# Chunked recurrence on one Trainium2 core: a new order of TensorE's groups within a chunk, a reordered prologue, and transfers that are merged, moved and split

## The chip, the cores and the metric

The kernel runs on one core of one Trainium2 chip. The metric is the device time of one execution in microseconds (us), here the median of several runs.

## The reference

Three parts follow one another: a recurrence over 768 steps for 4 batches x 8 heads with head dimension 40, a mixture of 8 experts (top 2), and a two-layer network. The change lies in the recurrence, and in the zeros that the routing needs in its sorted buffer.

```python
for t in range(S):                        # S = 768, state [B, H, 40, 40]
    y[:, :, t] = einsum('bhd,bhde->bhe', rt, state)
    Sa = einsum('bhde,bhe->bhd', state, at)
    state = state * wt[:, :, None, :] - einsum('bhd,bhe->bhde', Sa, bt)
    state = state + einsum('bhd,bhe->bhde', vt, kt)
x = attn_out as [3072, 320]
... top-2 routing: out[mask] += top2_w * (relu(x[mask] @ w1[e]) @ w2[e])
... h = x @ w_in; out = max(0.01 h, h) @ w_out
```

## The kernel before

The 768 steps are cut into 6 super-chunks of 128 steps (index s) and 24 chunks of 32 (index k = 4s + c, so c runs over 0 to 3). Everything of the recurrence is one unrolled program in `stage_a`, with the order of each engine written out by hand and semaphores between the engines. Stages for routing, experts and the last two layers follow and are not touched.

Per super-chunk: VectorE scans the reversed decays P to suffix products (`suffix`, L302) and the decays U to prefix products (`prefix`, L312); GpSimd multiplies A, B and K by them (`make_A`, `make_B`, `make_K`); TensorE forms two matrices per chunk, `lb` (L561) and `lk` (L571); ScalarE copies their diagonal blocks to LbS and LkT (`gram`). The LbS blocks go through DRAM (`lscr`) into lanes, Lt; VectorE solves a triangular system in 31 steps of a multiply (L331) and a reduction (L335), in `inverse`, a generator whose steps are spread over the chunks: 14 for c = 0, 12, 18, and the rest for c = 3. The result goes through DRAM (`tscr`) into TT. `decay` (L344) carries the state from one super-chunk to the next, behind the inverse in VectorE's order, and `y_out` (L357) of chunk k-2 stands ahead of chunk k's steps; it waits for p_y, which the last group of `add_K` raises.

Per chunk TensorE runs groups, in this order before: `first` (L533, X from the state), `gram_of(0)` (an `lk` or `lb` for a later super-chunk), `turn_S` (L599), `grow_K` (L632), `solve` (L609, needs TT), `gram_of(1)`, `read_S` in two halves (L623), `turn_P` (L614), `add_B` (L651), `tok`/`rows` (L582, L584 and L590, L592), `grow_B` and `add_K` in alternating halves (L642, L661), `gp` (L668), then for the next chunk `lkv` (L543) and `gv` (L554). `read_S`, `add_B` and `add_K` work on the output of the chunk before. ScalarE copies each result out of PSUM (its `copy` helper is L406): Xs, GvT, S0, PTs, Pn, S0T, Gpb; GpSimd masks GvT and Gpb.

SyncE's queue (SP) carries the wide inputs of a super-chunk (P, AT, BT, KT, each about 835 KB, `wide`), U (`decays`), and the ways through DRAM (`out_half`, `to_lanes`, `from_lanes`, `to_blocks`, the last with 16 transfers). ScalarE's queue loads each chunk's RT, VT and Vd two chunks ahead (`chunk`, six transfers) and stores the rows of the result. Vd is block-diagonal: its zeros are written once by GpSimd, each load fills four blocks of rows of 160 B. GpSimd starts one transfer of 9920 KB that fills `xsort` with zeros from xT (L273).

## Time and profile before

| | us |
|---|---|
| median of 3 runs | 1630.61 |
| lowest, highest | 1625.28, 1632.7 |
| the profiled execution, its own time | 1626.74 |
| its span in the trace | 1625.0 |
| TensorE busy (81%) | 1313.9 |
| VectorE busy (57%) | 921.0 |
| ScalarE busy (40%) | 653.4 |
| GpSimd busy (19%) | 315.4 |

The mean granted TensorE clock is 0.87 of full speed. In the trace an engine's busy time counts its compute instructions; "idle before" with an arrow names what ended the idle time, and "issue" means that the profile shows nothing that was waited for. Rows of a timeline begin with the start in us from the start of the span and the length.

### The profile page before, as it was taken

Reading aid. Unit: us, or ns where it says so; the run is one execution under the profiler, and the core shown is the slowest. Engines: PE = TensorE matmul, PEld = TensorE weight load, DVE = VectorE, ACT = ScalarE, POOL = GpSimd, SP = SyncE. Lnnn points to the kernel's source line nnn. Section 1 sums busy time; section 2 is a strip of 40 time slices with the busy share of each in tenths; the row PEclk is TensorE's granted clock in tenths of the full one; section 3 lists DMA queues with packets and bytes.
Section 4 is the critical chain, followed back from the end, with each engine's and each line's share of the span. In section 5 each row is a group of like instructions: output and inputs, shape, how many; then the busy total and the mean of one; then the engine's idle time right before and its main releaser. Section 6 shows DMA issues by size and latency. Waiting matters only on the chain. (4 is left out here: it accounts for less than half of the span.)

```text
span 1625.0 us, 40719 instructions
## 1 busy us (share of the span) xinstructions
PE 1313.9 (81%) x16814; PEld 1194.8 (74%) x16814; DVE 921.0 (57%) x1547; ACT 653.4 (40%) x1451; POOL 315.4 (19%) x255
## 2 busy tenths in 40 slices
PE   0546869798789895005999999999993999999998
PEld 0435758586677684005999999999993889889887
DVE  4575939555683502505777877777772453544533
ACT  0422434334344232204666666766661333323332
POOL 1332425241332110660000000000003210110000
PEclk9985877758687876557999999999996999999999
DMA  8577272624532212736667677677662110110000
GB/s 182 116 245 167 57 154 55 156 66 94 136 76 57 57 49 87 245 121 212 217 222 253 212 231 246 210 241 237 207 207 61 45 37 13 50 41 8 16 17 17
DMA packets 168287, 208.01 MB, mean 128 GB/s; under 512 B 86984, under 2 KB 138312, under 8 KB 164656
## 3 DMA queue, kind: packets, MB, share of 16 engines
q1 hardware_dynamic: 126532, 153.16, 32.5%
q0 software_dynamic: 9088, 36.05, 6.6%
q10 hardware_dynamic: 32540, 16.92, 4.2%
q8 instruction: 103, 1.69, 0.4%
q14 instruction: 24, 0.20, 0.0%
HBM read 163.75 MB, written 42.34 MB: 127 GB/s over the span
## 5 line engine op out<-in xcount | busy, mean ns | idle before, releaser
L331 DVE TENSOR_TENSOR prod<-Tl,Lt 128x1 f32<-128x1 f32 (+30 forms) x186 | 150.0, 807 | 40.1 <-DMA Lt<-lscr 33.9
L1241 DVE TENSOR_TENSOR gf<-psM,low 128x512 f32<-128x512 f32 x96 | 66.4, 691 | 179.0 <-ACT low L1279 179.0
L1084 PE MATMUL psE<-w2h,hh 128*128 128x320 f32 x496 | 155.7, 314 | 0.0
L1279 ACT ACTIVATE low<-psM 128x512 f32<-128x512 f32 x96 | 57.5, 599 | 242.2 <-PE psM L1337 242.2
L1086 PE MATMUL psE<-w2h,hl 128*128 128x320 f32 x496 | 153.3, 309 | 0.0
L1085 PE MATMUL psE<-w2l,hh 128*128 128x320 f32 x496 | 153.2, 309 | 0.0
L1069 PE MATMUL psE<-xh,w1h 128*128 128x256 f32 x496 | 141.2, 285 | 5.6 <-DVE w1l L974 5.6
L1070 PE MATMUL psE<-xl,w1h 128*128 128x256 f32 x496 | 141.1, 284 | 0.0
L1071 PE MATMUL psE<-xh,w1l 128*128 128x256 f32 x496 | 141.0, 284 | 0.0
L974 DVE TENSOR_TENSOR w2l<-w2t,w2h 128x320 fp32r<-128x320 f32 x248 | 122.2, 493 | 11.9 <-ACT w2h L969 11.9
L1316 PE MATMUL psM<-woh,gh 128*128 128x320 f32 x384 | 119.9, 312 | 2.9 <-DVE gl L974 2.3
L1141 DVE SCALAR_TENSOR_TENSOR hl<-psE,hh 128x256 fp32r<-128x256 f32 x248 | 105.3, 424 | 26.9 <-ACT hh L1110 3.6
L1318 PE MATMUL psM<-woh,gl 128*128 128x320 f32 x384 | 118.7, 309 | 0.0
L1317 PE MATMUL psM<-wol,gh 128*128 128x320 f32 x384 | 118.5, 309 | 0.0
L1110 ACT ACTIVATE hh<-psE 128x256 fp32r<-128x256 f32 x248 | 95.3, 384 | 53.3 <-PE psE L1073 52.1
L1156 POOL DMA_DIRECT2D ysort<-ys x31 | 22.3, 719 | 480.4 <-DVE ys L1148 480.4
L969 ACT ACTIVATE w2h<-w2t 128x320 fp32r<-128x320 f32 x248 | 114.8, 463 | 0.5
L974 DVE TENSOR_TENSOR w1l<-w1t,w1h 128x1024 fp32r<-128x1024 f32 (+1 forms) x93 | 108.1, 1218 | 2.1
L258 POOL TENSOR_TENSOR Gpb<-Gpb,neg_m 128x1024 f32<-128x1024 f32 x24 | 59.4, 2476 | 225.2 <-ACT Gpb L406 225.2
L1069 PEld LDWEIGHTS psE<-xh,w1h 128*128 128x128 f32 x496 | 95.9, 193 | 6.0 <-issue 6.0
L1051 PE MATMUL psE<-ident,xs 128*128 128x128 f32 x186 | 26.0, 277 | 89.7 <-DMA w1t<-in_w_dram 89.7
L335 DVE TENSOR_REDUCE Tl<-prod 128x1 f32<-128x1 f32 (+30 forms) x186 | 93.6, 503 | 5.8
(171 smaller groups left out, 3319.8 us busy)
## 6 DMA issues: line engine op xcount, KB each, us to landing
w2t<-in_w_dram SPq DMA_DIRECT2D x31, 1280.0 KB, 6.2
w1t<-in_w_dram SPq DMA_DIRECT2D x31, 1024.0 KB, 8.2
w1t<-in_w_dram SPq DMA_DIRECT2D x62, 256.0 KB, 8.6
xsort<-xT POOLq DMA_DIRECT2D x1, 9920.0 KB, 35.9
xs<-xsort SPq DMA_DIRECT2D x31, 320.0 KB, 5.7
ysort<-ys POOLq DMA_DIRECT2D x31, 320.0 KB, 4.1
P<-in_wR_dram SPq DMA_DIRECT2D x6, 838.5 KB
U<-in_wE_dram SPq DMA_DIRECT2D x6, 838.5 KB
```

The costliest lines, as they stand in the source:

```text
L331: mark(nc.vector.tensor_tensor(prod[:, 0:t, 0:t], Tl[:, 0:t, CH - t:CH], Lt[:, t:t + 1, CH - t:CH].to_broadcast([128, t, t]), ALU.mult))
L969: return nc.scalar.activation(hi, src, ACT.Copy)
L974: return nc.vector.tensor_tensor(lo, src, hi.bitcast(F32), ALU.subtract)
L1069: mm(o, w1h[:, j, fs], xh[:, p, j, :], start=(j == 0), stop=False)
L1070: mm(o, w1h[:, j, fs], xl[:, p, j, :], start=False, stop=False)
L1071: mm(o, w1l[:, j, fs], xh[:, p, j, :], start=False, stop=False)
L1084: mm(o, hh[:, f, sl], w2h[:, f, :], start=(f == 0), stop=False)
L1085: mm(o, hh[:, f, sl], w2l[:, f, :], start=False, stop=False)
L1086: m = mm(o, hl[:, f, sl], w2h[:, f, :], start=False, stop=(f == NF - 1))
L1316: mm(o, gh[:, f % 4, sl], woh[:, f, :], start=(f == 0), stop=False)
L1317: mm(o, gh[:, f % 4, sl], wol[:, f, :], start=False, stop=False)
L1318: m = mm(o, gl[:, f % 4, sl], woh[:, f, :], start=False, stop=(f == NF - 1))
```

## The change

- Prologue. P of super-chunk 0 is loaded in four pieces with a semaphore each, and each of the four suffix scans waits for its own piece; the scan's second input is `start`, set to ones at the four heads of its rows, and `fresh` is gone. The five constants are issued from ScalarE's queue. The lanes of super-chunk 0 are issued ahead of A, B, K of super-chunk 1 and of the first two chunks' loads. TensorE and ScalarE start without waiting for the last two memsets.
- Transfers. RT and VT become one tile RV; Vd comes from DRAM with its zeros in one transfer of 640 KB, and its memset is gone. P of super-chunk s+3 is issued at the end of c = 3 of s. The zeros of `xsort` come in 16 pieces on SP's queue, one after each of chunks 4 to 19.
- TensorE's order: `gv` moves from the end of the chunk before to behind `turn_P`, `gram_of(1)` from behind `solve` to behind `grow_B`, `read_S` is split around, and `add_K`'s second half stands behind `gp`. All grams of the loop use banks 6 and 7. ScalarE's order follows; Gpb's copy now stands ahead of the next loads' issue.
- VectorE: `prefix` comes at step 11 of c = 1, not 8.

TensorE in chunk 2 (c = 2), from a half of `grow_B` to the next chunk's `first`. Before, `grow_B` (L642) and `add_K` (L661) alternate, then `tok` (L582, L584), `gp` (L668), `lkv` (L543), `gv` (L554), `first` (L533):

```order
L642 MATMUL psA<-Pn,Bk 40x40 x16
L661 MATMUL psA<-GvT,Kk 40x32 x16
L642 MATMUL psA<-Pn,Bk 40x40 x16
L661 MATMUL psA<-GvT,Kk 40x32 x16
L582 MATMUL psA<-ident,BT 128x104 x4
L584 MATMUL psA<-ident,KT 128x104 x4
L668 MATMUL psA<-RT,PTs 128x128 x8
L543 MATMUL psA<-Vd,LkT 32x160 x8
L554 MATMUL psA<-RT,VT 32x32 x32
L533 MATMUL psA<-S0T,AT 32x40 x32
```

and with the change, from the second half of `grow_B` (now L639):

```order
L639 MATMUL psA<-Pn,Bk 40x40 x16
L562 MATMUL psA<-BT,AT 128x128 x8
L620 MATMUL psA<-RV,S 40x32 x16
L658 MATMUL psA<-GvT,Kk 40x32 x16
L579 MATMUL psA<-ident,BT 128x104 x4
L581 MATMUL psA<-ident,KT 128x104 x4
L665 MATMUL psA<-RV,PTs 128x128 x8
L658 MATMUL psA<-GvT,Kk 40x32 x16
L542 MATMUL psA<-Vd,LkT 32x160 x8
L532 MATMUL psA<-S0T,AT 32x40 x32
```

`gram_of(1)` (L562) and a half of `read_S` (L620) have moved in, `gv` has gone (it stands behind `turn_P` now), and the last half of `add_K` (L658) stands between `gp` (L665) and `lkv` (L542).

SyncE's queue at the start. Before:

```order
L166 DMA P<-in_wR_dram 104x2064
L167 DMA fresh<-in_cst_dram 104x516
L133 DMA U<-in_wE_dram 104x2064
L169 DMA BT<-in_bE_dram 104x2048
L170 DMA AT<-in_aE_dram 104x2048
L171 DMA ident<-in_cst_dram 128x128
L172 DMA triu<-in_cst_dram 128x128
L173 DMA neg_m<-in_cst_dram 128x128
L174 DMA pos_m<-in_cst_dram 128x32
L175 DMA wgn<-in_wgh_dram 104x64
L176 DMA KT<-in_kE_dram 104x2048
L133 DMA U<-in_wE_dram 104x2064
```

and with the change:

```order
L175 DMA P<-in_wR_dram 104x516 x4
L141 DMA U<-in_wE_dram 104x2064
L177 DMA BT<-in_bE_dram 104x2048
L178 DMA AT<-in_aE_dram 104x2048
L179 DMA KT<-in_kE_dram 104x2048
L141 DMA U<-in_wE_dram 104x2064
L147 DMA lscr<-LbS 128x512 x2
L155 DMA Lt<-lscr 32x32x32 x4
L127 DMA P<-in_wR_dram 104x2064
L185 DMA AT<-in_aE_dram 104x2048
L186 DMA BT<-in_bE_dram 104x2048
L187 DMA KT<-in_kE_dram 104x2048
```

The constants and `fresh` are gone from between P and KT, and the lanes (lscr, Lt) now stand ahead of AT, BT, KT of super-chunk 1 and of the first chunks' tiles.

The diff, cut to its core:

```diff
 def chunk(k):
-    sp.dma_start(RT[:, b3, :, :], rE[k]).then_inc(q[f"l_r{b3}"], 16)
-    sp.dma_start(VT[:, b2, :, :], vE[k]).then_inc(q[f"l_v{b2}"], 16)
-    for b in range(NB):
-        sp.dma_start(Vd[CH * b:CH * b + CH, b2, :, :, D * b:D * b + D], vG[k, b]).then_inc(q[f"l_g{b2}"], 16)
+    sp.dma_start(RV[:, b3, :, :, :], rvE[k]).then_inc(q[f"l_r{b3}"], 16)
+    sp.dma_start(Vd[:, b2, :, :, :], vG[k]).then_inc(q[f"l_g{b2}"], 16)
+def suffix_in(s):
+    sp.wait_ge(q["e_B"], 2 * s)
+    sp.wait_ge(q["e_K"], s)
+    sp.wait_ge(q["v_U"], 4 * s)
+    sp.wait_ge(q["v_end"], s)
+    sp.dma_start(P[:, :, :], wR[s]).then_inc(q["l_p"], 16)
+def zeros(j):
+    n = NTS * TS // 128
+    a, b = 4 * j, min(4 * j + 4, n)
+    sp.dma_start(xsort.rearrange("(n p) m -> p n m", p=128)[:, a:b, :],
+                 zer.rearrange("p (o m) -> p o m", o=1).to_broadcast([128, b - a, DM])).then_inc(q["l_zf"], 16)
 def wide(s):
-    sp.dma_start(P[:, :, :], wR[s]).then_inc(q["l_p"], 16)
...
                     to_blocks(s + 1)
+                    if s + 3 < NS_:
+                        suffix_in(s + 3)
+                if 4 <= k < 20:
+                    zeros(k - 4)
...
-            nc.gpsimd.memset(Vd[:, :, :, :, :], 0.0).then_inc(q["z_g"], 1)
+            nc.gpsimd.memset(TT[:, :, :, :, :], 0.0).then_inc(q["z_g"], 1)
...
 def suffix(s):
-    dve.wait_ge(q["l_p"], 16 * (s + 1))
+    if s:
+        dve.wait_ge(q["l_p"], 16 * s)
+        dve.wait_ge(q["v_U"], 4 * s)
+    mark(nc.vector.memset(start[:, 0:NB * (SC + 1):SC + 1], 1.0))
+    need()
     for h in range(4):
+        if s == 0:
+            dve.wait_ge(q[f"l_p{h}"], 16)
...
-            dve.wait_ge(q["l_c"], 96)
+            dve.wait_ge(q["z_v"], 2)
...
-                    if i == 8 and s + 2 < NS_:
-                        if c == 0:
-                            suffix(s + 2)
-                        if c == 1:
-                            prefix(s + 2)
+                    if c == 0 and i == 8 and s + 2 < NS_:
+                        suffix(s + 2)
+                    if c == 1 and i == 11 and s + 2 < NS_:
+                        prefix(s + 2)
...
                 copy(Xs[:, :, :, :].rearrange("p h b d -> p h (b d)"), ps[:, 4:6, 0:160], "a_X")
-                act.wait_ge(q["p_Gv"], k + 1)
-                copy(GvT[:, k % 2, :, :, :].rearrange("p h b t -> p (h b t)"), ps[:, 4, 256:512], "a_gv")
                 gram_of(0)
...
                 copy(flat(PTs[:, :, :]), ps[0:EP, 7, :], "a_PT")
-                gram_of(1)
...
+                act.wait_ge(q["p_Gv"], k + 1)
+                copy(GvT[:, k % 2, :, :, :].rearrange("p h b t -> p (h b t)"), ps[:, 4, 256:512], "a_gv")
...
+                gram_of(1)
...
-                if k + 2 < NK:
-                    chunk(k + 2)
                 act.wait_ge(q["p_Gp"], k + 1)
                 if k:
-                    act.wait_ge(q["p_y"], k)
+                    act.wait_ge(q["o_y"], 4 * k - 2)
                 copy(Gpb[:, :, :, :].rearrange("p (i x) h m -> p x i (h m)", x=2),
                      ps[:, 6:8, :].rearrange("p x (i m) -> p x i m", i=2), "a_Gp")
+                if k + 2 < NK:
+                    chunk(k + 2)
...
-                    pe.wait_ge(q["a_gv"], k + 1)
-                    gram_of(1)
...
                     read_S(k - 1, 0)
-                    pe.wait_ge(q["o_y"], 4 * k - 3)
-                    read_S(k - 1, 1)
+                    pe.wait_ge(q["g_gp"], k)
+                    add_B(k - 1)
                 if k < NK:
                     pe.wait_ge(q["a_PT"], k + 1)
                     turn_P()
...
+                    gv(k)
+                    pe.wait_ge(q["a_Pn"], k + 1)
+                    pe.wait_ge(q["o_S"], 2 * k + 1)
+                    grow_B(k, 0)
+                    pe.wait_ge(q["a_gv"], k + 1)
...
+                    pe.wait_ge(q["o_S"], 2 * k + 2)
+                    grow_B(k, 1)
+                    gram_of(1)
                 if k:
+                    pe.wait_ge(q["o_y"], 4 * k - 3)
+                    read_S(k - 1, 1)
                     pe.wait_ge(q["g_gv"], k)
                     pe.wait_ge(q["o_y"], 4 * k - 1)
                     add_K(k - 1, 0)
...
+                    pe.wait_ge(q["a_G"], before(k + 1))
+                    gp(k)
                 if k:
                     pe.wait_ge(q["o_y"], 4 * k)
                     add_K(k - 1, 1)
...
                     lkv(k + 1)
-                    gv(k + 1)
```

## Rows read from the trace of the kernel before

**Rows 1.** Windows, loop: us, busy (count) PE, PEld, DVE, ACT, POOL, clock, DMA share, GB/s

```profile
144.30:626.00 481.70, 408.82 (x10499) 339.68 (x10500) 273.52 (x391) 175.59 (x451) 152.59 (x97) 0.77 0.37 87
```

**Rows 2.** Timeline of the prologue: start us, length us, engine, instruction, idle before

```profile
24.11 4.61 DVE L304 TENSOR_TENSOR_SCAN P<-P,fresh 104x516 f32<-104x516 f32 x4 [18.26 <-DMA wgn<-in_wgh_dram]
...
35.02 6.10 POOL L229 TENSOR_TENSOR AT<-AT,U 104x1024 f32<-104x1024 f32 x2 [31.92 <-DVE U L318]
...
42.35 3.79 PE L564 MATMUL psA<-BT,AT 40*128 40x128 f32 x32 [42.35 <-DVE xT L373]
```

**Rows 3.** Timeline of chunk 0: last step of the inverse, then solve(0)

```profile
111.17 1.16 DVE L335 TENSOR_REDUCE Tl<-prod 128x31 f32<-128x961 f32 x1
...
131.09 1.94 PE L609 MATMUL psA<-TT,Xs 128*40 128x128 f32 x16 [28.28 <-DMA TT<-tscr]
```

**Rows 4.** The page's DMA issues: the fill; KB each, us to landing

```profile
xsort<-xT POOLq DMA_DIRECT2D x1, 9920.0 KB, 35.9
```

**Rows 5.** Timelines of SP, TensorE, VectorE at the boundary of chunks 3 and 4

```profile
200.47 0.32 SPq L153 DMA_DIRECT2D tscr<-Tl  x1
...
210.92 1.07 PE L609 MATMUL psA<-TT,Xs 128*40 128x128 f32 x16 [0.97 <-DMA TT<-tscr]
...
216.29 0.34 SPq L127 DMA_DIRECT2D P<-in_wR_dram  x1
...
223.49 5.94 DVE L304 TENSOR_TENSOR_SCAN P<-P,fresh 104x516 f32<-104x516 f32 x4 [13.66 <-DMA P<-in_wR_dram]
...
242.93 0.18 DVE L316 RECIPROCAL start<-P 104x4 f32<-104x4 f32 x1 [8.90 <-DMA U<-in_wE_dram]
```

**Rows 6.** Windows: the start, the burst of transfers, one load in a quiet stretch

```profile
24.00:30.00 6.00, 0.00 (x0) 0.00 (x0) 5.79 (x7) 0.00 (x0) 0.00 (x0) 1.00 0.84 191
...
216.00:242.00 26.00, 14.69 (x414) 12.35 (x416) 10.05 (x20) 6.92 (x16) 4.71 (x3) 0.67 0.81 191
366.00:372.00 6.00, 3.64 (x139) 2.77 (x136) 5.76 (x9) 1.92 (x5) 1.02 (x1) 1.00 0.43 101
```

**Rows 7.** Timelines of TensorE and VectorE around chunk 3 (c = 3)

```profile
179.74 0.50 PE L661 MATMUL psA<-GvT,Kk 32*40 32x32 f32 x31
...
180.28 0.69 DVE L357 TENSOR_TENSOR xT<-psA,U 104x512 f32<-104x512 f32 x1
...
183.84 0.77 PE L533 MATMUL psA<-S0T,AT 40*32 40x40 f32 x64 [0.27 <-PE psA L554]
...
200.36 0.81 DVE L344 TENSOR_TENSOR S0T<-psA,Wend 104x640 f32<-104x640 f32 x1
```

**Rows 8.** Windows: the c = 3 chunks 3, 7, 11, 15, 19, from first() to first()

```profile
183.84:201.34 17.50, 15.00 (x452) 12.55 (x453) 17.01 (x17) 7.48 (x19) 3.67 (x2) 0.90 0.18 48
...
273.28:291.34 18.06, 14.98 (x452) 12.29 (x452) 17.54 (x18) 7.84 (x20) 3.66 (x2) 0.91 0.25 67
...
369.25:389.01 19.76, 16.51 (x452) 13.69 (x453) 17.23 (x17) 7.59 (x19) 3.57 (x2) 0.83 0.22 61
...
460.45:477.85 17.40, 15.23 (x453) 12.54 (x453) 16.92 (x17) 7.48 (x19) 3.66 (x2) 0.90 0.20 46
...
539.25:556.28 17.03, 12.76 (x420) 10.51 (x421) 16.14 (x16) 4.59 (x11) 4.09 (x2) 0.90 0.20 53
```

**Rows 9.** Timeline of VectorE in chunk 19: y_out and decay

```profile
534.86 0.69 DVE L357 TENSOR_TENSOR xT<-psA,U 104x512 f32<-104x512 f32 x1 [4.20 <-PE psA L661]
...
554.43 0.82 DVE L344 TENSOR_TENSOR S0T<-psA,Wend 104x640 f32<-104x640 f32 x1
```

**Rows 10.** Timeline of VectorE in chunk 11: y_out

```profile
365.45 0.69 DVE L357 TENSOR_TENSOR xT<-psA,U 104x512 f32<-104x512 f32 x1 [6.11 <-PE psA L661]
```

**Rows 11.** Timeline of ScalarE's queue: one chunk's Vd loads

```profile
367.19 2.57 ACTq L441 DMA_DIRECT2D Vd<-in_vG_dram  x4
```

**Rows 12.** Groups of TensorE, 144 to 626 us: busy, mean ns, idle before

```profile
L574 PE MATMUL psA<-AT,KT 40*128 40x128 f32 x288 | 28.1, 346 | 9.9 <-issue 5.6 <-ACT Gpb L406 4.4
...
L564 PE MATMUL psA<-BT,AT 40*128 40x128 f32 x256 | 23.9, 336 | 5.9 <-ACT Gpb L406 5.9
```

More of the change, by code:

```diff
@@ L40, with stage_a @@
 KE = [(0, 128), (128, 128), (256, 64)]
-def stage_a(nc, st, wE, wR, aE, bE, kE, rE, vE, vG, cst, wgh, lscr, tscr, xrow, xsort):
+def stage_a(nc, st, wE, wR, aE, bE, kE, rvE, vG, cst, wgh, zer, lscr, tscr, xrow, xsort):
     ctx = ExitStack()
@@ L164, in to_blocks @@
                                      back[h, :, 8 * c:8 * c + 8, :]).then_inc(q[f"l_t{c}"], 16)
-            sp.dma_start(P[:, :, :], wR[0]).then_inc(q["l_p"], 16)
-            sp.dma_start(fresh[:, :], cst[0:EP, 416:416 + NB * (SC + 1)]).then_inc(q["l_c"], 16)
+            for h in range(4):
+                sp.dma_start(P[:, 4 * h:4 * h + 4, :], wR[0][:, 4 * h:4 * h + 4, :]).then_inc(q[f"l_p{h}"], 16)
             decays(0)
```

160 lines of the change are left out of this document (63 added, 97 removed).

## The prediction

> **What bounds the kernel now.** I read the busy time by stage first. The recurrence ends at 626 us, and its loop from first(1) on takes 481.70 of them [rows 1]; everything behind it (routing, experts, last two layers, 1625 - 626 = 999 us) has the same instructions before and after, so it is costed at nothing. In the loop TensorE is busy 408.82 us at a mean granted clock of 0.77, VectorE 273.52 us. That looks like a TensorE-bound loop, but the average hides a second chain, and the timeline shows it.
>
> Prologue: the first scan starts at 24.11 us, after 18.26 us of idle that ended with the arrival of wgn, the last of six small constants; the scan itself reads only P and `fresh` [rows 2]. The 35.02 row is the first product on GpSimd, the 42.35 row the first matmul, which waited for the xT memset.
>
> Chunk 0: the inverse of the first super-chunk is finished at 111.17 + 1.16 = 112.3 us, and solve(0), which needs it through `tscr` and TT, starts at 131.09 with 28.28 us of idle in front [rows 3]. Between them lies the fill of `xsort`, 9920 KB, 35.9 us to landing [rows 4].
>
> Stage boundary: super-chunk s+1's inverse lands at 200.47. The same SP queue then sends lanes and TT, so P goes out only at 216.29, the suffix scan waits 13.66 us for it, and U arrives for the prefix at 242.93 after another 8.90 us [rows 5]. From 216 to 242 the DMA engines are 0.81 busy at 191 GB/s [rows 6]: U lands when the queue has drained.
>
> Chunks with c = 3: TensorE ends add_K(k-2, 1) at 179.74 + 0.50, VectorE starts y_out at 180.28, then runs the rest of the inverse without a gap to 200.36, then the decay (0.81 us), and first() of the next chunk starts at 201.34 [rows 7, 8]. In that stretch VectorE is busy 17.01 of 17.50 us [rows 8]. The last such chunk looks alike (534.86 to 554.43) [rows 9]. So here VectorE, released by the end of add_K, is level with TensorE.
>
> **The change part by part.**
>
> 1. Start of VectorE. P comes in four pieces, no constant is waited for, and the constants go out on ACT's queue. Data ahead of the whole of P, U, BT and AT is then 3.35 MB plus 0.23 MB of constants. At 191 GB/s [rows 6] that is 18.7 us, with 3 to 4 us of start and landing 22 to 23 us for AT; the scans (4.61 us [rows 2], with the prefix 11 us up to the product) fit under it. make_A, at 35.02 before, starts near 23 and the first matmul near 26, against 42.35: **16 us** earlier. Bounds: 11 us, if the constants' queue slows P, and 18 us, the whole idle of the scan. AT, BT, KT for super-chunk 1 are now issued behind the first lanes; at the same rate they land some 13 us after that, before prefix(1) needs them, and the six tiles of chunks 0 and 1 behind them land before lkv(0). All of the prologue moves by the same 16 us.
>
> 2. The fill of `xsort` moves from one transfer in the prologue to 16 pieces of 640 KB on SP's queue during chunks 4 to 19. From the end of the inverse to solve took 131.09 - 112.3 = 18.8 us; at the next boundary, without the fill, it took 210.92 - 200.4 = 10.5 us [rows 5]. **8 us** more, bounds 4 and 9. Parts 1 and 2 give -24 us at solve(0), bounds -15 and -27.
>
> 3. add_K(k-1, 1) moves behind gp(k), just ahead of lkv(k+1). Before, y_out starts 183.84 - 180.28 = 3.6 us before the boundary [rows 7]; now only lkv stands between, so about 1.0 us. From y_out to the end of the decay takes 200.36 + 0.81 - 180.28 = 20.9 us, in the last stage 554.43 + 0.82 - 534.86 = 20.4 [rows 7, 9]; neither piece of work changed. A c = 3 chunk that is followed by a stage cannot be shorter than this less 1.0, so 19.4 to 19.9. The five took 17.50, 18.06, 19.76, 17.40 and 17.03, together 89.75 [rows 8]; five at 19.65 are 98.3. **+8.5 us**; bounds 0 (if TensorE is slower there anyway) and +12. The same lateness costs at TT: solve after the boundary must wait for the 10.5 us path, which before had slack at two of the boundaries: **+2**.
>
> 4. Transfers per chunk. RT and VT are one transfer, Vd is one of 640 KB with its zeros instead of four of 40 KB. A load in a quiet stretch moved 0.61 MB in 6 us at a mean share of 0.43, so 2.6 us of all engines, 235 GB/s of busy time [rows 6]; 0.48 MB more is 2 to 2.5 us at 235 to 191 GB/s. In the burst one such load, and one piece of zeros (0.66 MB, 3.4 us at the burst's rate), now stand before U; in the next two stages a second piece does. U is late by 6, 9 and 9 us. The prefix is also called three half steps later (about 1 us of wait covered). Stage 2 hides its delay: VectorE waited there for TensorE, 6.11 us in its c = 3 chunk [rows 10]. In stages 1 and 3 part 3 already holds the end back by some 2.5 us, which leaves 2.5 and 5.5; since the engines were only 0.81 busy in the burst, I take a third off. **+5 us**, bounds 0 and +16. P itself is not earlier: its new place, behind TT in the same queue, is where it physically stood. The cover of the moved fill is thus this queue's idle time; where there is none, U pays.
>
> 5. TensorE's order and ACT's. No matmul is added or removed. Gpb's copy stood behind the issue of the Vd loads (2.57 us [rows 11]); gram_of(0) waited for it 5.9 + 4.4 = 10.3 us in total [rows 12]. Now it precedes them and add_K and lkv lie between: the wait goes. What is late next is gp(k), which writes banks 6 and 7 and must wait until ACT has copied gram_of(1), now just ahead of it. gram_of(1) also opens GpSimd's make_A and make_B in c = 1. Half of the gain is in c = 3 chunks, which VectorE bounds. Between -10 and +4 I take **-4**.
>
> 6. At the end, add_B(23) has one read_S less before the mask: **+1**. The cleared Vd buffer, `fresh` and the end-of-GpSimd wait have no one waiting on them; the reset of `start` is four columns.
>
> Sum: -24 + 8.5 + 2 + 5 - 4 + 1 = -11.5 us. The profiled execution took 1626.7 us, which gives 1615; the median of the runs before is 1630.6, which gives 1619. I forecast **1617 us**.
>
> A part of the trace that has no term is the idle "issue" time in the middle of equal matmuls, such as 5.6 us before L574 [rows 12]; those gaps come while DMA is busy, and more bytes can make them longer. The Trainium skill, "Runtime: NRT & Kernel Launch", Instruction fetch mechanics, says that the sequencer fetches blocks of 256 instructions ahead and that this is mostly hidden; by it these gaps would not depend on the transfers, and the sum stays as it is. No row here says what the gaps are.
>
> **Rivals.**
>
> - The loop is neutral. VectorE was idle before c = 1, and the denser order may hold the full clock (mean 0.77 of it now); the 10.3 us are got back whole. For: TensorE has more work than VectorE. Against: the gapless 180.28 to 201.17. Time: 1626.7 - 24 = 1603.
> - The gain is eaten: parts 3 and 4 at their upper bounds, +12 and +12, cancel part 1 and 2. For: both chains are level now in four stages. Time: 1627 to 1631, no change.
> - Slower: U is so late that each of stages 1 to 3 is lengthened by its full lateness, because the moved pieces and Vd share the engines with the burst at half its rate. With 12 us in each, -24 + 8.5 + 2 - 4 + 1 + 36 = +19.5: 1646. It turns from gain to loss by more than 0.5% when U's term exceeds 25 us, over 8 us in each stage. For: U already lands with the last byte of the burst. Against: prefix's result is needed by gram_of in the next chunk only, and stage 2 has slack.
> - Vd's narrow rows cost more than their bytes, so the wide transfer is no dearer. Before, each Vd row piece is 160 B; the quiet load ran at 235 GB/s of busy time with them, no slower than the wide burst, which speaks against it. If it were so, part 4 would keep only the zeros: +2 instead of +5, so 1614. The Trainium skill, "DMA: Bandwidth & Descriptors", Specifications, says that transfers below 512 B do not reach line rate.
>
> **How the numbers follow.** Chances: forecast 0.45, neutral loop 0.25, gain eaten 0.17, slower 0.08, cheap Vd 0.05. What a measurement of this kernel can tell from no change is about 0.5%, 8 us, so the limits are 1622.5 and 1638.8. Faster: 0.38 of the forecast's 0.45, the neutral loop and cheap Vd, 0.68. Same: 0.07 + 0.17 = 0.24. Slower 0.08. The range runs from the neutral loop with the prologue's lower bound, 1600, past the eaten gain to 1634; it leaves out 0.08 below and 0.10 above.
>
> **What would show it.** Right: first scan near 6 us, first matmul near 26, solve(0) near 107; c = 3 chunks of 19.4 us and more with first() released by the decay; U arriving 6 to 9 us later after P; no wait for Gpb before gram_of(0). Wrong: c = 3 chunks of 17 us, a loop shorter than 475 us from first(1) to the end, or a first matmul later than 32.

## The result and the profile after

The change takes 1637.7 us (median of 20 runs, 1631.0 to 1648.7), the kernel before on the same chip 1624.2 us (20 runs). The ratio is 1.0068, with a 95% interval of 1.0046 to 1.0090: **slower**, by 11 us if one goes by the ratio (the two medians are 13.5 us apart), where I had forecast 1617 us and put 0.08 on slower. The profiled execution took 1636.8 us with a span of 1635.0; before it was 1626.7 and 1625.0. The difference between the two executions, +10.0 us of span, is what the rows below have to explain.

Timelines of VectorE and TensorE in the prologue of the change, to hold against [rows 2, 3]:

```profile
6.02 4.60 DVE L304 TENSOR_TENSOR_SCAN P<-P,start 104x516 f32<-104x516 f32 x4
12.69 1.23 DVE L318 TENSOR_TENSOR_SCAN U<-U,start 104x516 f32<-104x516 f32 x1
23.94 2.47 PE L562 MATMUL psA<-BT,AT 40*128 40x128 f32 x19 [23.94 <-DVE xT L370]
103.70 1.94 PE L606 MATMUL psA<-TT,Xs 128*40 128x128 f32 x16 [20.02 <-DMA TT<-tscr]
118.38 0.93 PE L532 MATMUL psA<-S0T,AT 40*32 40x40 f32 x64 [0.18 <-PE psA L542]
```

The scan starts 18.1 us earlier, the first matmul 18.4, solve(0) 27.4, and first(1) 25.9 us (118.38 against 144.30). The prologue brought what it should.

Windows of the change: the loop to its end, to hold against [rows 1], then the five c = 3 chunks, against [rows 8]. Columns: us, busy (count) of PE, PEld, DVE, ACT, POOL, granted clock, DMA share, GB/s.

```profile
118.38:631.93 513.55, 437.06 (x10561) 362.66 (x10561) 261.79 (x393) 177.76 (x450) 148.28 (x97) 0.73 0.45 121
...
158.60:179.57 20.97, 14.06 (x453) 11.69 (x453) 20.35 (x21) 7.69 (x19) 5.83 (x3) 0.95 0.40 119
253.28:275.39 22.11, 15.84 (x452) 12.96 (x452) 21.49 (x21) 7.69 (x19) 5.72 (x3) 0.80 0.45 132
346.10:367.07 20.97, 13.86 (x453) 11.73 (x453) 20.35 (x21) 7.69 (x19) 5.54 (x3) 0.88 0.48 141
443.83:466.10 22.27, 13.85 (x452) 11.50 (x453) 21.65 (x22) 7.69 (x19) 5.27 (x3) 0.96 0.46 139
528.67:548.68 20.01, 15.22 (x420) 12.10 (x420) 19.39 (x21) 4.70 (x11) 5.30 (x3) 0.77 0.27 79
```

The loop takes 513.55 us where it took 481.70: +31.9, of which TensorE's busy time is +28.2 (437.06 against 408.82), at a granted clock of 0.73 against 0.77 with the same matmuls. The rest of the program is 1635.0 - 631.9 = 1003.1 us against 999.0; nothing was changed there, and one execution of each does not tell 4 us from the spread of the runs. So -25.9 + 31.9 + 4.1 = +10.1.

The five c = 3 chunks take 106.3 us where they took 89.75. Timelines of chunk 3, against [rows 7]:

```profile
157.81 0.69 DVE L355 TENSOR_TENSOR xT<-psA,U 104x512 f32<-104x512 f32 x1 [0.37 <-PE psA L658]
...
173.31 0.75 PE L542 MATMUL psA<-Vd,LkT 128*32 128x160 f32 x16
...
178.70 0.81 DVE L344 TENSOR_TENSOR S0T<-psA,Wend 104x640 f32<-104x640 f32 x1
...
179.57 0.94 PE L532 MATMUL psA<-S0T,AT 40*32 40x40 f32 x64 [5.51 <-DVE S0T L344]
```

y_out starts 0.8 us before the boundary where it started 3.6 before, and from it to the end of the decay VectorE takes 21.7 us: TensorE is done with lkv at 174.06 and waits 5.51 us for the decay. Two groups of the whole loop (line, engine, op, tile, count, then busy us, mean ns, and the idle time before them):

```profile
L532 PE MATMUL psA<-S0T,AT 40*32 40x40 f32 x1472 | 21.6, 252 | 34.7 <-DVE S0T L344 22.7 <-issue 8.8 <-PE psA L542 3.2
L316 DVE RECIPROCAL start<-P 104x4 f32<-104x4 f32 x16 | 2.9, 180 | 39.1 <-DMA U<-in_wE_dram 38.7
```

first() waits 22.7 us for the decay (before: 1.4), and VectorE's prefix waits 38.7 us for U (before: 25.2). For Gpb nobody waits ahead of gram_of(0) any more. VectorE at the first boundary, against [rows 5]:

```profile
200.67 4.80 DVE L304 TENSOR_TENSOR_SCAN P<-P,start 104x516 f32<-104x516 f32 x4
...
224.58 0.18 DVE L316 RECIPROCAL start<-P 104x4 f32<-104x4 f32 x1 [13.86 <-DMA U<-in_wE_dram]
```

The other chunks show where the rest of the loss lies. These are sums over chunks 1 to 22, from first() to first(), of the two profiled executions (us; idle is the time less TensorE's busy time):

| chunks | before | busy | idle | clock | after | busy | idle | clock |
|---|---|---|---|---|---|---|---|---|
| five with c = 0 | 108.3 | 83.7 | 24.7 | .82 | 105.2 | 94.0 | 11.2 | .72 |
| six with c = 1 | 162.3 | 139.9 | 22.4 | .65 | 178.9 | 154.3 | 24.6 | .60 |
| six with c = 2 | 103.5 | 96.7 | 6.7 | .78 | 102.2 | 98.6 | 3.7 | .80 |
| five with c = 3 | 89.8 | 74.5 | 15.3 | .89 | 106.3 | 72.8 | 33.5 | .87 |

The c = 3 chunks are longer by idle time alone, and most of that comes back as less idle time in the c = 0 chunks behind them. What remains is busy time at a lower clock, in the chunks with c = 0 and c = 1.

### The profile page after: what moved, and what is told of

Its sections match the earlier page's. It is cut to its first block and busy times, and to the rows that moved or that the text cites. A ratio compares the mean times of both kernels' runs of the same rounds, so it can differ in the third digit from the quotient of the medians.

```text
span 1635.0 us, 40604 instructions
## 1 busy us (share of the span) xinstructions
PE 1341.4 (82%) x16814; PEld 1217.7 (74%) x16814; DVE 909.5 (56%) x1553; ACT 655.1 (40%) x1451; POOL 304.8 (19%) x253
## 5 line engine op out<-in xcount | busy, mean ns | idle before, releaser
L331 DVE TENSOR_TENSOR prod<-Tl,Lt 128x1 f32<-128x1 f32 (+30 forms) x186 | 142.9, 768 | 38.0 <-DMA Lt<-lscr 31.9
L355 DVE TENSOR_TENSOR xT<-psA,U 104x512 f32<-104x512 f32 x24 | 16.5, 689 | 144.2 <-PE psA L658 144.2
```

The lines of the kernel that those rows point to most:

```text
L331: mark(nc.vector.tensor_tensor(prod[:, 0:t, 0:t], Tl[:, 0:t, CH - t:CH], Lt[:, t:t + 1, CH - t:CH].to_broadcast([128, t, t]), ALU.mult))
```

## The experiments

Every kernel was run 5 to 12 times, next to the kernel before on the same chip. To compare the loops at one place in all of them, I read each profile from first(1) to first(23), all but the last chunk. These windows, one of each kernel's, carry most of what follows:

Kernel before:
```profile
144.30:608.13 463.83, 394.75 (x10021) 328.12 (x10022) 272.13 (x389) 171.90 (x444) 147.91 (x95) 0.77 0.39 90
```
The change:
```profile
118.38:611.07 492.69, 419.74 (x10021) 348.30 (x10021) 260.41 (x391) 173.96 (x443) 143.82 (x95) 0.73 0.47 126
```

| kernel | ratio [95% interval] | loop us | PE busy us | clock | busy x clock | idle us | of it for the decay |
|---|---|---|---|---|---|---|---|
| before | 1 | 463.8 | 394.8 | .77 | 304 | 69 | 1 |
| change | 1.0068 [1.0046, 1.0090] | 492.7 | 419.7 | .73 | 306 | 73 | 23 |
| e1 old order | 0.9949 [0.9916, 0.9983] | 470.5 | 392.8 | .77 | 302 | 78 | 8 |
| e2 new order alone | 1.0170 [1.0135, 1.0206] | 482.6 | 418.0 | .73 | 305 | 65 | 18 |
| e3 add_K early | 1.0079 [1.0047, 1.0112] | 484.2 | 417.7 | .74 | 309 | 66 | 14 |
| e4 interleaved | 1.0217 [1.0182, 1.0253] | 518.4 | 450.0 | .66 | 297 | 68 | 0 |
| e5 = e1, fill late | 0.9937 [0.9914, 0.9960] | 481.2 | 395.8 | .76 | 301 | 85 | 8 |
| e6 = e1, narrow Vd | 0.9884 [0.9848, 0.9921] | 466.5 | 394.6 | .76 | 300 | 72 | 8 |
| e7 lkv repeated | 1.0097 [1.0060, 1.0135] | 500.8 | 427.7 | .74 | 316 | 73 | 7 |
| e8 gv back | 1.0175 [1.0137, 1.0212] | 504.0 | 432.1 | .71 | 307 | 72 | 1 |
| e9 gv, gram_of(1) back | 1.0150 [1.0110, 1.0190] | 517.0 | 441.2 | .69 | 304 | 76 | 5 |
| e10 = e6, fill late | 0.9859 [0.9828, 0.9891] | 466.8 | 396.2 | .75 | 297 | 71 | 10 |
| e11 change, narrow Vd | 1.0025 [1.0003, 1.0046] | 487.4 | 414.0 | .73 | 302 | 73 | 28 |
| e12 = e10, prefix early | 0.9903 [0.9865, 0.9940] | 474.9 | 394.8 | .76 | 300 | 80 | 14 |
| e13 = e10, add_K late | 0.9899 [0.9863, 0.9935] | 460.4 | 386.4 | .78 | 301 | 74 | 25 |
| e15 = e10, grow_B in a row | 0.9928 [0.9897, 0.9960] | 478.4 | 402.7 | .76 | 306 | 76 | 12 |
| e16 = e10, read_S split | 0.9984 [0.9953, 1.0015] | 493.1 | 411.8 | .74 | 305 | 81 | 5 |
| e17 = e10, gv late | 0.9976 [0.9949, 1.0003] | 472.1 | 404.4 | .75 | 303 | 68 | 14 |
| e18 = e11, read_S whole | 1.0014 [0.9988, 1.0040] | 488.8 | 413.7 | .74 | 306 | 75 | 14 |
| e19 = e18, add_B between | 1.0039 [0.9997, 1.0081] | 493.8 | 425.9 | .73 | 311 | 68 | 7 |

The profile is one execution, the ratio many, and one kernel's executions lie up to 29 us apart: the profiled one of e1 took 1610.1 us (median 1619.9), of e3 1630.6 (1640.5), of e13 1597.2 (1604.8), of e17 1610.4 (1620.5), of e5 1621.7 (1614.5). Where a row and a ratio differ by some microseconds, the ratio decides.

The clock doesn't rest on one execution. Every execution lists the mean granted clock of its whole span, loop and rest. The kernel before has .870 to .874 as a mean on each of the five chips, the change .852 (20 executions, .846 to .858). With the old order, e1 has .868 (12, .859 to .874) and e10 .870 (5, .866 to .876); with the new order, e2 has .857 (6, .854 to .862) and e11 .855 (12, .852 to .859); the slowest mixture, e4, has .837 (6, .830 to .843).

**e1 and e2: order against everything else.** e1 is the change with TensorE's and ScalarE's order of before, but with Gpb's copy still ahead of the next loads; e2 is the kernel before with the new order alone. The core of e1's edit (e2's is the reverse, on the other kernel):

```diff
                     solve(k)
+                    gram_of(1)
...
                     read_S(k - 1, 0)
-                    add_B(k - 1)
+                    read_S(k - 1, 1)
                     turn_P()
-                    gv(k)
+                    add_B(k - 1)
                     grow_B(k, 0)
-                    grow_B(k, 1)
-                    gram_of(1)
-                    read_S(k - 1, 1)
                     add_K(k - 1, 0)
+                    grow_B(k, 1)
+                    add_K(k - 1, 1)
                     gp(k)
-                    add_K(k - 1, 1)
                     lkv(k + 1)
+                    gv(k + 1)
```

> The change with TensorE's and ScalarE's order of the loop put back (Gpb's copy stays ahead of the next loads' issue), with the new prologue, transfers and fill. Theory 1 (clock: the new order puts the narrow matmuls in one long run, the granted clock drops to 1.2 GHz, busy time in the loop rises by 28 us) and theory 2 (VectorE is released late by add_K in the c = 3 chunks) both expect the whole prologue gain, some 25 us: 1600 us, ratio 0.985, TensorE busy in the loop near 409 us. Theory 3 (the wider Vd, the zeros and the later U cost the 28 us) expects no better than the change, 1630 to 1638.

> The kernel before with the new order of TensorE and ScalarE in the loop alone. Theories 1 and 2: the loop's loss without the prologue's gain, 1650 to 1665 us, ratio 1.02. Theory 3: 1615 to 1630, no slower than before.

```profile
115.94:586.42 470.48, 392.81 (x10020) 326.90 (x10021) 270.15 (x392) 172.80 (x443) 148.22 (x95) 0.77 0.50 133
```
This is e1; e2 below.
```profile
145.65:628.22 482.57, 418.03 (x10020) 344.16 (x10021) 266.81 (x388) 172.65 (x443) 142.56 (x95) 0.73 0.37 86
```

The new order costs 1.7 points alone, 28 us, and 1.2 on top of the rest (1.0068 - 0.9949, 19 us). Its cost is TensorE's busy time: +23.3 us in e2 against before, +26.9 in the change against e1, and 5 us less idle time both times. Prologue and transfers without the order gain 0.5 points, 8 us, of the 26 that the prologue brought. So e1 lies between what the theories expected of it (1600, or 1630 to 1638): the order is the larger loss, and the rest of the change has one too.

**e3: the late add_K.** The change with both halves of add_K(k-1) ahead of gp(k):

```diff
                     add_K(k - 1, 0)
+                    pe.wait_ge(q["o_y"], 4 * k)
+                    add_K(k - 1, 1)
                 ...
                     gp(k)
-                if k:
-                    pe.wait_ge(q["o_y"], 4 * k)
-                    add_K(k - 1, 1)
```

> The change with the second half of add_K put back ahead of gp, everything else as changed. Theory 2: y_out starts some 2 us earlier in each chunk, the waits of first() for the decay (22.7 us in the five c = 3 chunks) shrink by 2 us or more each, and the clock is kept: 1615 to 1620 us. Theory 1: the run of narrow matmuls is as long as before, 1630 to 1637 us, busy time in the loop still near 437 us.

The c = 3 chunks fell from 106.3 to 94.4 us, so the late add_K is what lengthens them; and the kernel is no faster, 1.0079 against 1.0068. The five c = 0 chunks behind them went from 105.2 to 110.6 us. The loop of this one execution is 8.5 us shorter than the change's, but it is among the fastest of its twelve. The wait for the decay was there, and it was not the price.

**e4: pieces of the old order between the new.** The change with read_S whole and grow_B and add_K alternating again; gv and gram_of(1) stay late.

```diff
                     read_S(k - 1, 0)
+                    read_S(k - 1, 1)
                     add_B(k - 1)
                     turn_P()
                     gv(k)
                     grow_B(k, 0)
+                    add_K(k - 1, 0)
                     grow_B(k, 1)
+                    add_K(k - 1, 1)
                     gram_of(1)
-                    read_S(k - 1, 1)
-                    add_K(k - 1, 0)
                     gp(k)
-                    add_K(k - 1, 1)
```

> The change with both halves of read_S together again and the halves of grow_B and add_K alternating again; gv stays behind turn_P and gram_of(1) behind the growth of the state. Theory 1, in the form that the separated halves of grow_B and add_K make the narrow run: busy time in the loop falls to near 410 us, 1600 to 1612 us. Theory 1, in the form that gv and the late gram_of(1) make it: still 1625 to 1637 us. Theory 2: as the kernel with add_K early, 1615 to 1620.

1.0217, slower than any of the theories had it. gp and solve wait here for what comes late (line, busy, idle before):

```profile
L665 PE MATMUL psA<-RV,PTs 40*128 40x128 f32 x352 | 44.0, 422 | 17.3 <-ACT LbS L402 8.3 <-ACT LkT L402 8.2 <-issue 0.6
...
L606 PE MATMUL psA<-TT,Xs 128*40 128x128 f32 x352 | 29.4, 322 | 11.4 <-DMA TT<-tscr 11.4
```

gram_of(1) stands directly ahead of gp, which needs its bank; the clock falls to 0.66. A mixture is not the sum of its pieces.

**e5 and e6: the transfers, on e1.** e5 puts the zeros two per chunk into chunks 16 to 23; e6 brings back Vd's narrow load:

```diff
-                if 4 <= k < 20:
-                    zeros(k - 4)
+                if k >= 16:
+                    sp.wait_ge(q["p_X"], k)
+                    zeros(2 * k - 32)
+                    zeros(2 * k - 31)
```
```diff
-                sp.dma_start(Vd[:, b2, :, :, :], vG[k]).then_inc(q[f"l_g{b2}"], 16)
+                for b in range(NB):
+                    sp.dma_start(Vd[CH * b:CH * b + CH, b2, :, :, D * b:D * b + D], vG[k, b]).then_inc(q[f"l_g{b2}"], 16)
```

> The kernel with the old order and the new prologue (first experiment: 1619.9 us, ratio 0.995), but the 16 pieces of zeros two per chunk in chunks 16 to 23, where no wide inputs are loaded, instead of one in each of chunks 4 to 19. If the zeros in the bursts cost (U later, longer gaps without a named wait, 54 us of them in the loop there): 1605 to 1612 us, ratio near 0.99. If the wider Vd costs and not the zeros: 1617 to 1622.

> The same kernel with old order and new prologue, but Vd again loaded without its zeros in four transfers of 160-byte rows per chunk, with the buffer cleared once. If the wider Vd's bytes cost: 1605 to 1612 us. If the narrow rows are the dearer ones, or ScalarE's longer issue: 1622 to 1630. If neither: 1617 to 1622.

The zeros cost nothing that can be told (0.9937 against 0.9949, 2 us; e5's 1614.5 us lie between what the two theories had). The wide Vd costs 0.65 points, 10 us; the two intervals just overlap, and e10 and e11 below show the same with 13 and 7 us. The DMA views of both loops, e1 first (queue: packets, MB, share of 16 engines; tile: count, KB, median us to landing):

```profile
q10 hardware_dynamic: 8600, 26.96, 20.1%
...
Vd<-in_vG_dram ACTq DMA_DIRECT2D x21, 640.0 KB, 6.3
```
```profile
q10 hardware_dynamic: 29255, 16.24, 15.3%
...
Vd<-in_vG_dram ACTq DMA_DIRECT2D x85, 40.0 KB, 3.9
```

Four times 40 KB in rows of 160 B, with 3.4 times the packets of the queue, take the engines less time than 640 KB in wide rows.

**e7: is it idle time that costs the clock?** The change with lkv run four times in c = 3, in the wait for the decay; the repeats write the same values.

```diff
-                    lkv(k + 1)
+                    lkv(k + 1, 4 if c == 3 else 1)
```

> The change, but in c = 3 chunks the eight products of lkv(k+1) are run four times over with the same result, in the time in which first() waits for the decay (1.7 to 5.6 us, 22.7 in sum). If the half clock behind the boundary is due to this idle time, the c = 0 chunks begin at the full clock and get 2 to 4 us shorter each: 1622 to 1630 us. If the clock has fallen already in the narrow run ahead of it, nothing: 1635 to 1640.

1.0097 against 1.0068. The wait for the decay shrinks from 23 to 7 us, but the repeats are no free filling: the five c = 3 chunks grew from 106.3 to 116.8 us, and the c = 0 chunks behind them got 3.0 us shorter together, where 2 to 4 us each had been expected. The mean clock of the whole execution is .859 (6, .856 to .862) against .852 in the change, with work added. So filling this gap buys no time; that the idle time has some part in the clock is not excluded.

**e8 and e9: gv and gram_of(1).** The change with gv(k+1) behind lkv(k+1) again; e9 moves gram_of(1) back behind solve(k) as well. This is e9's edit, e8's has the lines of gv alone:

```diff
                     solve(k)
+                    gram_of(1)
...
                     turn_P()
-                    gv(k)
...
                     grow_B(k, 1)
-                    gram_of(1)
...
                     lkv(k + 1)
+                    gv(k + 1)
```

> The change with gv alone put back behind lkv (64 narrow matmuls fewer in the run from turn_P to add_K). Clock theory: the run is 0.8 us shorter, the clock falls there in fewer chunks, busy time in the loop falls from 437 towards 420 us: 1622 to 1630 us. VectorE theory: add_K is 0.8 us earlier against the boundary, the waits shrink but the chunks do not: 1633 to 1640.

> The change with two of its moved groups back where they were: gv(k+1) behind lkv(k+1), and gram_of(1) behind solve(k), with its two alternating banks. What stays of the new order: read_S in two halves, both halves of grow_B ahead of add_K, the second half of add_K behind gp. The same chip time with gv alone back was 1.0175 of the kernel before, the change itself 1.0068. If the late gram_of(1) is the costly piece (it lengthens the row of groups with few rows behind turn_P, in which the granted clock falls): PE busy of the stretch from first(1) to first(23) falls from 419.7 us towards 395, its clock rises from .73 to .76 or more, and the ratio is 0.995 to 1.000. If the row of groups that are left (grow_B, read_S, add_K, gp, add_K) does it: busy time stays above 410 us, and the ratio is 1.008 to 1.018.

1.0175 and 1.0150, both slower than the change; e8 is also slower than either theory had it. e9 asked whether the late gram_of(1) is the costly piece: it is not, since busy time rose to 441 us without it. What is left of the new order in e9 (add_B ahead of turn_P, the split read_S, the two halves of grow_B in a row, the late add_K) costs 2 points against e1.

**e10, e11, e12: the best combination, and two cross-checks.** e10 is e6 with the late fill, e11 the change with only the narrow Vd, e12 is e10 with prefix three half steps earlier, as before.

```diff
-                    if c == 1 and i == 11 and s + 2 < NS_:
+                    if c == 1 and i == 8 and s + 2 < NS_:
```

> What the two runs of the parts suggest together: the change with the order of TensorE and ScalarE of before (0.9949 alone), narrow Vd transfers in four pieces on the old pattern (0.9884 with it), and the zeros of xsort issued two per chunk in chunks 16 to 23 (0.9937 against 0.9949, a difference within its interval). If transfers beside the loop are what ate the gain of the prologue, 0.986 to 0.989, that is 1600 to 1605 us against 1622; if the fill costs nothing wherever it lies, the same 0.988 as without it. Theory of the transfers falls if it comes out above 0.993.

> The change as it is, new order included, with only the Vd transfer narrow again (four pieces per chunk, buffer cleared by GpSimd once). With the old order that was worth 0.6 points (0.9949 to 0.9884). If transfers and order cost independently, 1.0068 falls to about 1.000 (some 1626 us on a chip where the kernel before takes 1626), with the c = 3 chunks still near 20 us and PE busy of first(1) to first(23) near 418 us. If the new order hides the wide transfer (the idle time before instructions, 29 us against 54 with the old order, is already small in it), the ratio stays at 1.005 to 1.009.

> e10 with one edit on VectorE: prefix(s+2) at step 8 of the inverse in c = 1 again instead of step 11. It tests the term of the prediction that put +5 us on rows that come later. If VectorE waits there for U, which its trace shows 6 to 9 us later than before, the inverse ends later and to_lanes with it: 1 to 4 us slower than e10, with a wait of the scan on the U transfer. If the cushion of the three steps was never needed, no difference within 0.2%.

e10 has the lowest ratio measured, 1605.5 us against 1629.2, with an interval that overlaps e6's. Between it and e11, which differ in the order and in the place of the fill, lie 1.7 points, as in e2. In the change the narrow Vd is worth 0.4 points, 7 us; between e5 and e10, which differ in it alone, 0.8 points, 13 us. The late fill (e6 to e10) is worth 0.25 points, inside the intervals. e12 came out 0.4 points above e10, more than either theory said, with overlapping intervals: the earlier prefix gains nothing, and whether it costs is open. (U is 3 to 4.5 us later in the change, not the 6 to 9 that the expectation of e12 names; see below.)

**e13, e15, e16, e17: one move of the new order at a time, on e10.**

```diff
-                    add_K(k - 1, 1)
                 gp(k)
+                    add_K(k - 1, 1)
```
is e13. In e15, e16 and e17:
```diff
                     grow_B(k, 0)
+                    grow_B(k, 1)
                     add_K(k - 1, 0)
-                    grow_B(k, 1)
                     add_K(k - 1, 1)
```
```diff
                     read_S(k - 1, 0)
-                    read_S(k - 1, 1)
...
                     grow_B(k, 0)
+                    read_S(k - 1, 1)
```
```diff
                     add_B(k - 1)
+                    gv(k)
+                    grow_B(k, 0)
                     tok(s + 1, TOKS[c][0])
-                    grow_B(k, 0)
...
                     lkv(k + 1)
-                    gv(k + 1)
```

> e10 (0.9859 of the kernel before) with one move of the new order: the second half of add_K(k-1) behind gp(k), and Gpb's copy waiting for add_B alone. The prediction priced it at +8.5 us in the five c = 3 chunks and +2 at the boundary, since VectorE reads y later. If it does that here: 0.992 to 0.993, with c = 3 chunks of 20 us where e10 has 16.6 to 20.7. If TensorE merely does other work ahead of the same wait, within 0.2% of e10.

> e10 with one move: both halves of grow_B(k) in a row, ahead of both halves of add_K(k-1). S0T's copy then starts some 1 us earlier in c = 0 to 2 and decay in c = 3; in return add_K ends later and y_out with it. Theory of the clock (a row of groups with few rows lowers it): PE busy from first(1) to first(23) rises from 396 us by 5 or more, ratio 0.99 or above. Theory of the waits: no rise of busy time, 0 to -3 us.

> e10 with one move: the second half of read_S(k-1) behind grow_B(k, 0) in place of directly behind the first half. turn_P then comes about 1 us earlier behind solve, so that the wait for PTs' copy is less covered. If it is that cover which counts, TensorE waits for PTs at turn_P (0.5 us a chunk, +10 us, 0.992); if it is the clock, busy time up from 396 us without a new wait; if neither, 0.984 to 0.988.

> e10 with one move: gv(k) behind add_B(k-1) in place of behind lkv(k), its copy to GvT behind Pn's, and the first token or row group behind grow_B(k, 0), since it needs gv's bank. In the change, putting gv back cost 1.1 points, so gv's new place should gain: first(k+1) comes 0.9 us earlier behind lkv in 23 chunks. If independent of the rest, 0.976 to 0.981. If the place behind turn_P lengthens the row of narrow groups and with it lowers the clock, busy time rises by 5 us or more and the ratio is 0.99 or above.

Against 0.9859: +0.4, +0.7, +1.25 and +1.2 points; e16 is above all that was expected of it. In e17, gv adds onto what gram_of(1) left in its bank, so the values differ, the instructions don't. All four moves go the wrong way or nowhere, and their sum, 3.5 points, is twice what the whole order costs. Two more moves of the new order, gram_of(1) behind grow_B and add_B ahead of turn_P, were not tried alone. e13 and e16, in that order:

```profile
115.97:576.39 460.42, 386.39 (x10020) 322.07 (x10021) 268.38 (x392) 172.01 (x443) 142.82 (x95) 0.78 0.46 113
```
```profile
116.53:609.67 493.14, 411.81 (x10020) 341.42 (x10021) 259.49 (x392) 172.09 (x443) 141.31 (x95) 0.74 0.45 105
```

e13 waits 25.1 us for the decay, more than the change, and the loop of its profiled execution, the fastest of seven, is the shortest of all. e16 hardly waits for it at all (5.2) and its loop is 26 us longer than e10's. So the wait that I had priced does not tell the time here.

**e18 and e19: the dearest move out of the change, and a test of the row of narrow groups.** e18 is e11 with read_S whole; e19 also has add_B behind grow_B(k, 1).

```diff
                     read_S(k - 1, 0)
+                    read_S(k - 1, 1)
-                    add_B(k - 1)
                     turn_P()
                     gv(k)
                     grow_B(k, 0)
                     grow_B(k, 1)
+                    add_B(k - 1)
                     gram_of(1)
-                    read_S(k - 1, 1)
```

> e11 (the change with narrow Vd, 1.0025) with the second half of read_S(k-1) directly behind the first again, the rest of the new order as it is. If the split costs here what it cost alone on the old order (0.9859 to 0.9984), 0.990 and a busy time of first(1) to first(23) of some 402 us where e11 has 414. If the pieces don't add and every mixture is as slow as the whole, 1.000 to 1.008.

> e18 with add_B(k-1), the group of 128 rows and 128 columns, moved from ahead of turn_P to behind grow_B(k, 1), so that the narrow groups from gv to gp don't stand in one row. Theory of the clock: mean granted clock of first(1) to first(23) rises by .01 or more against e18, and busy time falls by 5 us or more; but turn_P then waits some 0.5 us a chunk for PTs' copy, which add_B had covered (+10 us of wait). Without an effect of the row on the clock: busy time as in e18, and the ratio 0.5 points above it.

e18: 1.0014 against 1.0025, no difference; what the split costs on the old order it doesn't cost in the new one. e19: a wide group between the narrow ones raised neither the clock (.73) nor lowered the busy time (426 against 414). The theory that a row of narrow groups lowers the clock is thus not borne out in the new order: e8, e9 and e19 each break up or shorten that row and are no faster. In the old order e15 and e17 came out as it said (busy time up by 6.6 and 8.3 us, 0.9928 and 0.9976). It can't be the whole cause; more isn't shown.

## Why the prediction was wrong

Its sign was wrong because of one step, part 5, which put the reordering at -4 us. Part 4 was too small as well.

- **Parts 1 and 2, right.** -24 us at solve(0) predicted, -27.4 measured, just past the bound of -27, and -25.9 at first(1); first scan 6.02 (6), first matmul 23.94 (26), solve(0) 103.70 (107).
- **Part 3, right in place, wrong as a price.** c = 3 chunks of 19.4 us and more, released by the decay: 20.0 to 22.3, five of them +16.6 us where I had +8.5. But taking the late add_K out (e3) gave the chunks back 12 us and the kernel nothing, and putting it in alone (e13) cost 0.4 points, with intervals that overlap e10's. I had added a stage's lengthening to the sum as if the stages after it kept their lengths. They don't: in the change the c = 3 chunks have 18.2 us more idle time and the c = 0 chunks behind them 13.5 us less.
- **Part 4, too small.** +5 predicted. The profiled execution of e1 has +6.7 us in the loop, all of it idle time, but it is the second fastest of twelve. By the ratio e1 gains 8 us where the prologue brings 26, so the rest of the change without the order costs some 18 us (an estimate from the two; e1's interval is 5 us to either side), and 15 of them go in e10, with the narrow Vd and the late fill. I had the wrong weight inside it: the wide Vd is 7 to 13 us and the zeros 0 to 4. The first prefix of chunk 5 starts 23.9 us after the scan of P, before it was 19.4 us [rows 5], so U is 4.5 us later, not 6; in the next two stages it is 3.4 and 3.1 us later (22.9 for 19.6, 23.3 for 20.2), not 9.
- **Part 5, the step that failed.** "TensorE's order and ACT's. No matmul is added or removed... Between -10 and +4 I take -4." Only waits were in it. The waits did as it said: none for Gpb, and 4.2 us in all ahead of gp for the copy of gram_of(1). What I left out is that the same 10,021 matmuls take other times in another order: 394.8 us at a mean clock of 0.77, 419.7 us at 0.73. The remark in a rival that "the denser order may hold the full clock" shows that the clock was thought of, as a gain only. Measured, the order costs +19 us on top of the rest (e1), +28 alone (e2).
- Part 6 can't be told apart at this size.

By the ratios the measured +11 us splits into -26 + 18 + 19: prologue, the rest without the order, and the order. In the three profiled executions the same reads -26 + 7 + 22 to first(23), and +7 more in the last chunk and the unchanged rest: +10; e1's fast execution moves some of the 18 into the 22.

Of the rivals, the slower one came in, but not by its mechanism. It had U's lateness of 12 us in three stages; U was late by 3.1 to 4.5, and the same transfers with the old order make a faster kernel. The rival "cheap Vd" is refuted from the other side: narrow rows are not dearer but cheaper here. The neutral loop rested on "the denser order may hold the full clock"; the order is denser (idle 65 against 69 us, e2 against before), and the clock is lower. The gaps that the prediction left without a term did not grow with the bytes: gaps of 1.5 us and more with no named wait add up to 34.8 us before, 35.6 in e1 and 19.5 in the change; the last section has what they are.

**What the loss is made of.** In the table, busy time times clock stays at 297 to 311 us in every version that doesn't add work: at full clock the loop would be some 303 us of matmul, an estimate from these products. The idle time is 65 to 85 us and doesn't sort the kernels. What sorts them, roughly, is the clock that this work got. Shown is that the order sets it, by intervention in both directions (e1 against the change, e2 against before), and in the means over all their executions. The experiments move TensorE's groups and ScalarE's copies together, so they don't tell the two apart. Not shown is by what. The Trainium skill, "TensorE: Matmul & The Clock Gate", Part 1, has the level go by how busy TensorE has been. By the rows that alone doesn't tell these two apart: TensorE is busy for 394.75 / 463.83 = 85.1% of the loop before and 419.74 / 492.69 = 85.2% of it after, at .77 and .73. That is a mean over the loop, though, and doesn't speak of shorter stretches.

One stretch shows what such a loss looks like. Windows of 3 us of the change in chunk 5 (columns as above), and TensorE's timeline there:

```profile
198.00:199.20 1.20, 1.04 (x19) 0.46 (x20) 0.00 (x0) 0.59 (x1) 0.53 (x1) 0.56 0.91 184
199.20:202.20 3.00, 0.32 (x6) 0.15 (x6) 1.59 (x3) 0.00 (x0) 1.81 (x1) 0.50 1.02 245
202.20:205.20 3.00, 0.12 (x14) 0.12 (x22) 3.00 (x3) 0.00 (x0) 0.00 (x0) 0.50 0.93 205
...
208.20:211.20 3.00, 3.00 (x22) 2.34 (x22) 2.24 (x9) 2.19 (x5) 0.00 (x0) 0.50 0.91 208
...
214.20:217.20 3.00, 2.67 (x117) 2.17 (x109) 0.00 (x0) 0.88 (x3) 0.19 (x1) 1.00 0.83 215
217.20:220.20 3.00, 2.46 (x23) 2.41 (x23) 0.00 (x0) 0.26 (x2) 1.22 (x2) 0.74 0.91 299
220.20:223.20 3.00, 3.00 (x45) 2.89 (x45) 0.00 (x0) 0.89 (x6) 0.00 (x0) 0.50 0.82 198
...
220.00:242.00 22.00, 21.64 (x316) 19.07 (x317) 13.72 (x16) 8.27 (x24) 12.62 (x6) 0.50 0.42 129
```
```profile
199.16 0.35 PE L532 MATMUL psA<-S0T,AT 40*32 40x40 f32 x6 [0.16 <-PE psA L542]
205.08 0.89 PE L532 MATMUL psA<-S0T,AT 40*32 40x40 f32 x58 [5.57 <-issue]
...
217.74 0.28 PE L639 MATMUL psA<-Pn,Bk 32*40 32x40 f32 x8 [0.87 <-issue]
...
219.74 0.94 PE L587 MATMUL psA<-ident,xT 104*128 104x104 f32 x4
220.47 1.77 PE L589 MATMUL psA<-wgn,xT 104*128 104x16 f32 x8
```

The granted clock falls to 0.50 (1.2 GHz) at about 198, ahead of the gap of 5.57 us, and stays there until about 211.8; it is full (2.4 GHz) to about 218.6, and 0.50 again past the end of the chunk at 235.45, though TensorE is busy for 21.64 of the 22 us from 220 to 242. So a TensorE that the trace shows busy does not bring the full clock back here. The row groups run in that second part: three of the four groups of eight L589 matmuls take 1.77 us, the first 1.53. The kernel before in the same chunk:

```profile
238.50:241.50 3.00, 3.00 (x66) 2.53 (x65) 0.00 (x0) 0.74 (x2) 0.00 (x0) 0.91 0.74 166
241.50:244.50 3.00, 2.91 (x87) 2.44 (x76) 1.54 (x2) 1.86 (x6) 0.73 (x1) 1.00 0.07 16
244.50:247.50 3.00, 3.00 (x139) 2.97 (x142) 2.86 (x5) 1.15 (x6) 0.00 (x0) 1.00 0.15 55
247.50:250.50 3.00, 3.00 (x50) 2.96 (x40) 2.90 (x5) 1.28 (x4) 1.12 (x1) 0.80 0.18 60
```
```profile
244.20 0.98 PE L592 MATMUL psA<-wgn,xT 104*128 104x16 f32 x8
...
249.38 1.77 PE L592 MATMUL psA<-wgn,xT 104*128 104x16 f32 x8
```

The clock is full from 239 to about 249.5; three of the four groups take 0.98 us, only the last 1.77. Nothing in the change makes row groups dearer; they moved from a stretch of full clock into one of half. Over the loop their 160 matmuls take 25.5 us before and 30.4 after.

## What to carry to other kernels

When only the order of an engine's work changes, do not price it by its waits alone. Multiply TensorE's busy time by its granted clock before and after: if the product stands still and the busy time doesn't, the loss is clock, and no wait in the trace will account for it. Look at the clock of several executions, since single ones lie up to 17 us from their median here. And a stage's new wait is not a price until the stages behind it have been read too: here the execution with the shortest loop has 25 us of it, and in the change most of the new wait comes back as less waiting in the next chunk. A pure reordering that looks neutral is best measured separately from the changes that it comes with; the new prologue with the old order, the narrow Vd and the late fill is 1.4% faster than the kernel before (0.9859), and the reordering and the wide Vd hid that.

## What the runs showed of the hardware

- Zeros that are loaded along with data cost more than narrow rows: 640 KB in 6.3 us at 20.1% of the engines for the queue, against four times 40 KB in 160-B rows (3.9 us each) at 15.3%; 7 to 13 us of kernel time in three pairs of kernels (e1 and e6, the change and e11, e5 and e10).
- TensorE stops in the middle of equal, released matmuls. In the loop before there are ten such gaps of 1.5 us and more, 34.8 us together, and in six of them the DMA engines are 83% busy or more; in e1 ten with 35.6, in the change seven with 19.5, of which three lie where the DMA engines are that busy. In chunk 5 both kernels have one of 5.57 us, at other instructions (before ahead of the second matmul of L574 [rows 12], after ahead of the seventh of L532). They are gaps in the delivery of instructions, by their times: the trace has a DMA queue of the kind "instruction", with 79 packets of 16 KB in the loop, and in all 27 gaps of the three executions TensorE goes on 1.3 to 1.9 us after such a packet has ended. At a moment picked at random that would be so in about one case in eight (both worked out from the packets' times in the traces). For the gap before from 227.98 to 233.55, the queue's line is found in the stretch 230.70 to 232.10 and neither in the one ahead of it nor in the one behind; for the gap after, in 202.30 to 203.70 (packets, MB, share of the engines; before, then after):

```profile
q8 instruction: 1, 0.02, 5.7%
```
```profile
q8 instruction: 1, 0.02, 5.8%
```

  In the longest gaps the packet starts only 2 to 4 us into the gap. Why it comes so late there isn't shown: the DMA engines are 83% busy or more in all gaps over 5 us, but the change moves more bytes than before and has the smaller sum of gaps. The Trainium skill, "Runtime: NRT & Kernel Launch", Instruction fetch mechanics, says that fetching is hidden behind issue. By these rows it is hidden for most of the 79 packets and not for ten of them, 7% of the loop before.
- A TensorE that is busy without a gap can stay at the half clock: 21.64 busy us of 22 at 0.50 in chunks 5 and 6 of the change.
- Which order gets the higher clock could not be predicted from the rows, nor from the runs: all mixtures of the two orders that I tried on the change are as slow as the new order or slower, up to 1.0217.
